# The experts' first product by a Strassen scheme on two of the three channel blocks, with VectorE adding the products up

## The reference

```python
# y: result of a linear recurrence over 768 steps (attention part), as (3072 tokens, 384)
h = y @ w_in                     # 384 -> 2048
g = where(h >= 1, h, where(h <= -1, 0, (h + 1)**2 / 4))
x = g @ w_out                    # 2048 -> 384
P = exp(x @ w_gate - max)        # 3072 tokens x 8 experts
for _ in range(8):               # Sinkhorn: rows, then columns
    P /= P.sum(1) + 1e-9; P /= P.sum(0) + 1e-9; P *= N / E
out = 0
for e in range(8):
    h = maximum(x @ w1[e], 0)    # 384 -> 1024
    out += P[:, e:e+1] * (h @ w2[e])   # 1024 -> 384
```

## Time and profile before

| | |
|---|---|
| median of 3 runs | 2408.18 us (2406.64 to 2408.28) |
| the profiled execution | 2405.71 us, its span 2403.9 us |
| PE busy | 2293.7 us, 95% of the span |
| VectorE busy | 1032.8 us, 43% |
| ScalarE busy | 763.2 us, 32% |
| GpSimd busy | 327.4 us, 14% |
| experts' stage | from 795.1 us to the end |
| second product (L1254 to L1256) | 4608 matmuls of 384 columns |
| first product (L1138 to L1140, tile w_h) | 3456 matmuls of 512 columns |
| mean DMA rate | 44 GB/s |

### The profile page before, as it was taken

How to read it: one execution, slowest core, us unless ns; L and a number is a source line. 1 busy time by engine, 2 the same in 40 slices (tenths; PEclk the granted TensorE clock), 3 DMA queues, 4 the chain that set the end, 5 groups by cost and what they waited for, 6 DMA issues and landing times.

```text
span 2403.9 us, 36292 instructions
## 1 busy us (share of the span) xinstructions
PE 2293.7 (95%) x14011; PEld 2138.7 (89%) x14011; DVE 1032.8 (43%) x2075; ACT 763.2 (32%) x1519; POOL 327.4 (14%) x421
## 2 busy tenths in 40 slices
PE   2689999999999999999999999999999999999999
PEld 2689999999999889999998999999999899999998
DVE  6888888888873343222222222222222222222222
ACT  3455555555545212221122211222112221122211
POOL 0000000000002212111111111111111111111100
PEclk9799999999999999999999999999999999999999
DMA  3211111111111301101111111141011111011101
GB/s 105 83 40 50 50 51 48 48 48 47 48 34 58 132 29 36 36 30 29 31 36 36 29 29 31 36 153 30 30 31 36 36 31 29 29 36 35 29 14 27
DMA packets 95411, 106.63 MB, mean 44 GB/s; under 512 B 9448, under 2 KB 89576, under 8 KB 95208
## 3 DMA queue, kind: packets, MB, share of 16 engines
q1 hardware_dynamic: 95208, 103.99, 14.1%
HBM read 89.80 MB, written 14.16 MB: 43 GB/s over the span
## 4 chain that ended last, share of the span: by engine, by line
PE 82%; DVE 8%; ACT 7%; issue 2%; DMA 1%; SPq 0%; POOL 0%; ACTq 0%; DVEq 0%
PE bank L1138 14%; PE bank L1139 13%; PE bank L1140 13%; PE bank L1254 11%; PE bank L1256 11%; PE bank L1255 11%; PE bank L1119 2%; PE bank L1125 2%; PE bank L1124 2%; PE bank L1129 1%; ACT ubuf L561 1%; ACT ubuf L563 1%; ACT ubuf L559 1%; PE bank L1114 1%; DVE tmp L712 1%
## 5 line engine op out<-in xcount | busy, mean ns | idle before, releaser
L658 ACT ACTIVATE h_h<-bank 128x512 fp32r<-128x512 f32 x384 | 229.5, 598 | 1246.2 <-PE bank L1140 1236.1
L1254 PE MATMUL bank<-w_h,h_h 128*128 128x384 f32 x1536 | 516.4, 336 | 0.0
L1256 PE MATMUL bank<-w_h,h_l 128*128 128x384 f32 x1536 | 516.2, 336 | 0.0
L1255 PE MATMUL bank<-w_l,h_h 128*128 128x384 f32 x1536 | 516.1, 336 | 0.0
L989 DVE SCALAR_TENSOR_TENSOR h_l<-bank,h_h 128x512 fp32r<-128x512 f32 x384 | 264.6, 691 | 519.7 <-ACT h_h L658 519.3
L487 POOL TENSOR_TENSOR w_l<-stage,w_h 128x256 fp32r<-128x256 f32 x384 | 285.0, 744 | 1292.2 <-ACT w_h L639 1292.1
L1138 PE MATMUL bank<-x2h,w_h 128*128 128x512 f32 x1152 | 451.5, 392 | 2.6 <-issue 2.3
L1139 PE MATMUL bank<-x2l,w_h 128*128 128x512 f32 x1152 | 451.7, 392 | 0.0
L1140 PE MATMUL bank<-x2h,w_l 128*128 128x512 f32 x1152 | 448.9, 390 | 0.0
L1002 DVE SCALAR_TENSOR_TENSOR acc<-bank,prob,acc 128x384 f32<-128x384 f32 x168 | 103.9, 618 | 578.9 <-PE bank L1256 578.9
L1254 PEld LDWEIGHTS bank<-w_h,h_h 128*128 128x128 f32 x1536 | 288.1, 188 | 1.9
(11 more groups left out here) (135 smaller groups left out, 2741.4 us busy)
## 6 DMA issues: line engine op xcount, KB each, us to landing
stage<-w_ SPq DMA_DIRECT2D x384, 128.0 KB, 2.1
qb<-q_in_ SPq DMA_DIRECT2D x24, 192.0 KB
kb<-k_in_ SPq DMA_DIRECT2D x24, 192.0 KB
vb<-v_in_ SPq DMA_DIRECT2D x24, 192.0 KB
x_hi<-x2h_s SPq DMA_DIRECT2D x36, 128.0 KB, 1.8
x_lo<-x2l_s SPq DMA_DIRECT2D x36, 128.0 KB, 1.8
x2h<-x_hi SPq DMA_DIRECT2D x6, 768.0 KB, 8.2
x2l<-x_lo SPq DMA_DIRECT2D x6, 768.0 KB, 9.7
```

The costliest lines, as they stand in the source:

```text
L658: act.activation(h_h[:, f], hc[f % 3][:], ACT.Relu).then_inc(hh_done, 1)
L1254: pe.matmul(dst, h_h[:, f, t_], w2s[slot][0][:, f], start=f == 0, stop=False)
L1255: pe.matmul(dst, h_h[:, f, t_], w2s[slot][1][:, f], start=False, stop=False)
L1256: mm = pe.matmul(dst, h_l[:, f, t_], w2s[slot][0][:, f], start=False, stop=f == NF2 - 1)
```

## The change

The first product of the experts, h = x @ w1, is computed block by block. In each half q of the hidden dimension (four tiles) two of the three channel blocks are multiplied by a Strassen-Winograd scheme of two by two blocks; the tokens of a chunk are cut into two columns of 256. It takes seven products where the plain form takes eight; the third channel block takes its plain four, added in the same banks. That makes 11 block products per half, each two tiles by 256 tokens. The banks then hold partial products that have to be added: VectorE makes seven sums per half (`add`, from `p1_s`, `u2_s`, `u4_s`, `u3_s`), three of them to SBUF and four back into the bank. ScalarE copies p1 to SBUF (`keep_p1`), and the Relu and low part read the summed banks.

The scheme needs sums of weight blocks (S_1 to S_4) and of token blocks (T_1 to T_4, D_3). VectorE makes them from the raw tiles (`w1_sums`, `xt_sums`), ScalarE rounds them, and VectorE makes all low parts of w1 and x2's sums (`w1_lo`, `xt_lo`). GpSimd keeps only w2's low parts, in four pieces of 768 elements.

The tokens are taken in three passes of two chunks, not two of three, so that each expert's weights are loaded three times. w1 has one buffer in two halves and two staging tiles; w2 has two buffers. The y banks are two instead of four, and the y block's tiles come in the order 2, 3, 0, 1. The Sinkhorn rounds are cut into `sink_rows` and `sink_columns` and placed in the first two groups. `gate` of the last group stands behind the first four products of group 0. In the tail ahead of the experts VectorE and ScalarE also build the first weights and the first chunk's sums.

```diff
-            expert_lo(0, 0, 0, PER_E)
-            expert_lo(1, 1, 0, PER_E)
+            w2_lo(0, 0)
...
+            def xt_sums(ps, j):
...
+                dve.wait_ge(x2_in[j], 32 * (ps + 1))
+                for a, b in ((T_1, X_11), (T_3, T_3), (T_2, X_22), (T_4, X_21)):
+                    dve.tensor_tensor(to[:, a], high[:, b], low[:, b], ALU.add).then_inc(xt_sum, 1)
...
+            def w1_sums(ex, q):
...
+                dve.tensor_tensor(to[:, S_1], raw_[:, 0, :, 1], raw_[:, 1, :, 1], ALU.add).then_inc(w1_sum, 1)
+                dve.tensor_tensor(to[:, S_3], raw_[:, 0, :, 0], raw_[:, 0, :, 1], ALU.subtract).then_inc(w1_sum, 1)
...
+            def w1_lo(ex, q):
...
+                dve.tensor_tensor(w1l[:, q, W_11:W_22], raw_[:, :, :, 0], w1h[:, q, W_11:W_22].bitcast(F32),
+                                  ALU.subtract).then_inc(w1_low, 1)
...
+                if m == 1:
+                    w1_sums(0, 0)
+                    xt_sums(0, 0)
+                if m == 2:
+                    w1_lo(0, 0)
+                if m == 4:
+                    xt_lo(0, 0)
+                    w1_sums(0, 1)
+                if m == 6:
+                    w1_lo(0, 1)
...
+            def add(g, name, product, kept):
+
+                n = g * len(SUM)
+                q = int(name[3])
+                dve.wait_ge(h2_step, g * len(H2) + H2[product])
+                if name[:2] == "u2":
+                    dve.wait_ge(p1_kept, g * 2 + q + 1)
+                else:
+                    dve.wait_ge(sum_done, n + SUM[{"u4": "u2", "u3": "u2", "22": "u3", "12": "u4", "11": "u2",
+                                                   "21": "u3"}[name[:2]] + name[2:]])
+                dve.tensor_tensor(group_sum(name), pairs_of(h_bank[product]), kept[:], ALU.add).then_inc(sum_done, 1)
...
+            def group(ex, j, ps, e, nxt, x2_next):
+                g = ex * GP + j
+                first, second = (isinstance(g, int) and g == i for i in range(2))
+                build = nxt and j == 1
+                if second:
+                    sink_rows(4)
+                sums(g, 0, ("u2", "u4", "u3", "22", "12"))
+                if second:
+                    sink_columns(4)
+                h_lo(g, "22_0")
+                sums(g, 0, ("11",))
+                h_lo(g, "12_0")
+                if first:
+                    gate_out(GROUPS - 1)
+                    gate_max(0)
+                sums(g, 0, ("21",))
+                h_lo(g, "11_0")
+                if second:
+                    sink_rows(5)
+                sums(g, 1, ("u2",))
+                h_lo(g, "21_0")
...
+                h_lo(g, "11_1")
+                h_lo(g, "21_1")
+                if first:
+                    sink_rows(0)
+                if second:
+                    sink_rows(6)
+                if build:
+                    w1_sums(ex + 1, 0)
+                for k in range(B):
+                    if first:
+                        sink_columns(k)
+                        if k < 3:
+                            sink_rows(k + 1)
+                    if second and k < 2:
+                        sink_columns(6 + k)
+                        if k == 0:
+                            sink_rows(7)
+                    if build and k < 2:
+                        w1_lo(ex + 1, k)
+                    if build and k == 0:
+                        w1_sums(ex + 1, 1)
+                    add_expert(g, j, k, ps, e)
+                    if x2_next and k == 2:
+                        xt_sums(*x2_next)
+                if x2_next:
+                    xt_lo(*x2_next)
...
+            def product(name, j, terms):
+
+                q = int(name[3])
+                for i in range(2):
+                    to = h_bank[name][:, i * HT:(i + 1) * HT]
+                    for n, (w, x) in enumerate(terms):
+                        mm = three(to, (w1h[:, q, w, i], w1l[:, q, w, i]), (x2s[j][0][:, x], x2s[j][1][:, x]),
+                                   n == 0, n == len(terms) - 1)
+                mm.then_inc(h2_step, 1)
...
+                if first:
+                    pe.wait_ge(xt_low, 2 * (ps * GP + j + 1))
+                if not zero:
+                    pe.wait_ge(sum_done, back + SUM["u3_1"])
+                product("p1_0", j, ((W_11, X_11),))
+                if not zero:
+                    pe.wait_ge(hl_done, (g - 1) * len(LOW) + LOW["12_1"])
+                product("p6_0", j, ((S_2, T_2),))
+                product("p5_0", j, ((S_1, T_1),))
+                if not zero:
+                    pe.wait_ge(hl_done, (g - 1) * len(LOW) + LOW["11_1"])
+                product("p7_0", j, ((S_3, T_3), (W_23, X_32)))
+                if zero:
+                    pe.wait_ge(x2l_done, KT * GROUPS)
+                    pe.wait_ge(lg_done, GROUPS - 1)
+                    gate(GROUPS - 1)
+                else:
+                    pe.wait_ge(hl_done, g * len(LOW))
+                if one:
+                    sum_of_columns(4)
+                product("12_0", j, ((S_4, X_22), (W_13, X_32)))
+                pe.wait_ge(p1_kept, g * 2 + 1)
+                product("11_0", j, ((W_12, X_21), (W_13, X_31)))
+                pe.wait_ge(sum_done, here + SUM["u2_0"])
+                product("21_0", j, ((W_22, T_4), (W_23, D_3)))
...
+                pe.wait_ge(sum_done, here + SUM["u3_0"])
+                product("p1_1", j, ((W_11, X_11),))
+                pe.wait_ge(hl_done, g * len(LOW) + LOW["12_0"])
+                product("p6_1", j, ((S_2, T_2),))
...
+                for k, m in enumerate(M_ORDER):
+                    if k >= 2:
+                        pe.wait_ge(acc_done, g * B + k - 1)
...
+                        if n == 4 and (zero or one and k < 2):
+                            sum_of_columns(k if zero else 6 + k)
```

More of the change, by code:

```diff
@@ L378, in _ @@
+            for j in range(GP):
+                sp.wait_ge(out_done[j], PASSES * 16 * B)
         @block.gpsimd
@@ L670, in _, with keep_p1 @@
-            for hf in range(2):
-                e0 = E * hf
-                expert(e0, 0, True)
+            def keep_p1(g, q):
+                act.wait_ge(h2_step, g * len(H2) + H2[f"p1_{q}"])
+                if q:
+                    act.wait_ge(sum_done, g * len(SUM) + SUM["11_0"])
+                elif not isinstance(g, int) or g:
+                    act.wait_ge(sum_done, (g - 1) * len(SUM) + SUM["11_1"])
+                act.activation(p1_s[:], pairs_of(h_bank[f"p1_{q}"]), ACT.Copy).then_inc(p1_kept, 1)
@@ L673, in _, with expert @@
+            def expert(ex, slot, ps, last=False):
+                for j in range(GP):
+                    zero = isinstance(ex, int) and ex == 0
+                    x2_next = (0, 1) if zero and j == 0 else (ps + 1, j) if last and ps + 1 < PASSES else False
+                    group(ex, j, slot, zero and j == 0, not last or ps + 1 < PASSES, x2_next)
+            for ps in range(PASSES):
+                e0 = E * ps
+                expert(e0, 0, ps)
                 with act.Fori(0, 3) as r:
-                    expert(e0 + 1 + 2 * r, 1, True)
@@ new lines, in sums, with h_lo @@
+            def sums(g, q, names):
+                product = {"u2": "p6", "u4": "p5", "u3": "p7", "22": "p5", "12": "12", "11": "11", "21": "21"}
+                kept = {"u2": p1_s, "u4": u2_s, "u3": u2_s, "22": u3_s, "12": u4_s, "11": p1_s, "21": u3_s}
+                for n in names:
+                    add(g, f"{n}_{q}", f"{product[n]}_{q}", kept[n])
+            def h_lo(g, name):
+                dve.wait_ge(hh_done, g * len(SPLIT) + SPLIT[name])
+                dve.scalar_tensor_tensor(tiles_of(h_l, name), group_sum(name), 0.0, tiles_of(h_h, name).bitcast(F32),
@@ new lines, in expert @@
+            def expert(ex, ps, e, last=False):
+                for j in range(GP):
+                    zero = isinstance(ex, int) and ex == 0
+                    x2_next = (0, 1) if zero and j == 0 else (ps + 1, j) if last and ps + 1 < PASSES else False
+                    group(ex, j, ps, e, not last or ps + 1 < PASSES, x2_next)
+            for ps in range(PASSES):
+                e0 = E * ps
+                expert(e0, ps, None)
+                if ps == 0:
+                    for i in range(GP * B):
+                        j, m = i // B, M_ORDER[i % B]
+                        dve.wait_ge(acc_done, i + 1)
+                        dve.tensor_scalar(acc[:, j * B + m], acc[:, j * B + m], prob[:, j * B + m, 0:1], None, ALU.mult)\
+                           .then_inc(scaled, 1)
+                    dve.wait_ge(scaled, GP * B)
@@ L1219, in expert_block, with sum_of_columns, h_block @@
+            def sum_of_columns(r):
+                pe.wait_ge(sink, 3 + 9 * r + 5)
+                pe.matmul(sk[:, 0:E], ones[:], cold[:], start=True, stop=True).then_inc(sink_pe, 1)
+            def h_block(ex, j, ps, first):
+                g = ex * GP + j
+                zero, one = (isinstance(g, int) and g == i for i in range(2))
```

(10 more changed lines are left out.)

498 lines of the change are left out of this document (305 added, 193 removed).

## The result

| | before | after |
|---|---|---|
| median of 4 runs each | 2408.23 us (2406.64 to 2408.81) | 2392.72 us (2389.88 to 2393.52) |
| ratio | | 0.9935, interval 0.9917 to 0.9952 |
| profiled execution, its span | 2405.71, 2403.9 us | 2392.51, 2390.7 us |
| experts' third group (group 2) starts at | 866.23 us | 884.19 us |

The change saves 15.5 us. I had forecast 2380 us, a gain of 28. Group 2 here is the third of the 48 groups, counted from 0: the first after both opening groups. From it to the last matmul lie 46 groups, in both kernels. Before they took 2399.3 - 866.2 = 1533.1 us, after 2386.0 - 884.2 = 1501.8. So the steady part gives 31.3 us, and the start takes 18.0 back: 13.3 us together, as the spans say (2403.9 - 2390.7 = 13.2). The other 2 us of the medians lie outside the spans.

The account below looks back on a forecast made before the run. TensorE's stream of columns was taken to bound the experts' stage. 880.1 + 46 x 32.13 (1478.0) + 5 + 3 + 5 + tail 4.6 gave a 2375.7 us span, forecast as 2380 us, range 2354 to 2410 (8 in 10).

Parts of the forecast that it names:

- case (d): Whole kernel: TensorE sets the time, with only short stalls, as forecast at 2380 us; chance 0.65.
- third tile: Second y block of each expert: third tile waits for the first accumulation, booked at 0.2 us x 24 experts, 5 us.
- Part 1: Experts' h block: 132 matmuls of 256 columns at 116 ns, 15.31 us; a group 32.13 us, 1.16 less.
- Rival (c): Experts' blocks: 256 columns always cost 118 ns and y 177: +18 us, 2398, still faster; chance 0.10.
- Part 2: Experts' h block: VectorE's sums and low parts finish about 0.5 us before TensorE needs them; no stall booked.
- Rival (a): Experts' h block: VectorE sets the pace; at 0.83 us per operation TensorE waits 48 us, 2428, slower; chance 0.13.
- Part 3: Second y block of each expert: VectorE's weight build delays TensorE by 0.2 us x 24 experts, 5 us (0 to 24).
- Rival (b): Third y tile: the weight build holds it up in full, 1 us x 24: +19 us, about 2401; chance 0.12.
- Part 5: Experts' loop, three passes for two: nine loop edges, not six, cost 5 us; x2's sums cost 3 us.
- Passes: Pass changes: x2's sums end 3.7 us into the next h block, 0.8 us of stall, 4 times, 3 us.
- Part 4: Opening two groups: 18 us of stalls, group 0 starting at 793.5 us and group 2 at 880.1, not 866.2.
- theory A: Forecast for e4: matmul pace depends on both operands lying in upper memory, so even groups stay at 120 ns.

Follow-up runs that it names:

- e1: Kernel before the change, each 512-column matmul of the experts' first product cut into two of 256 columns: 2436.61 us, ratio 1.0117.
- e7: Changed kernel, second and third matmul of each triple of the first product cut from 256 to 128 columns, leaving out some low-part terms: 2381.0 us, one run.
- e5: Changed kernel with one more, unused VectorE sum of 512 elements in the first half of every group: 2399.89 us, one run.
- e6: Changed kernel with two more, unused VectorE sums of 512 elements in the first half of every group: 2441.93 us, one run.
- e3: Changed kernel with VectorE's first y accumulation moved ahead of the second half's weight sums: 2389.55 us, ratio 0.9917.
- e2: Changed kernel with the loops over the middle experts written out on all five engines: 2380.32 us, ratio 0.9885.
- e9: Changed kernel with GpSimd starting the second expert's w2 low parts only after the seventh Sinkhorn round: 2394.06 us, ratio 0.9945.
- e4: Changed kernel with the first chunk's x2 buffer laid 43,008 bytes per partition higher, same instructions: 2392.42 us, one run.

## Why the prediction was right in kind and short in size

The time fell inside the range and on the side forecast, by the mechanism forecast, the forecast's case (d). The gain was 15.5 us, not 28. The predicted span was 2375.7 us and the measured one 2390.7, so the sum was 15.0 us short. Term by term, over 46 groups:

```
h block     (15.686 - 15.312) x 46                        +17.2
y block     (16.645 - 16.82) x 46                          -8.0
third tile  0.18 x 23 for 5 booked                         -0.9
loop edges  9.8 for 5 booked                               +4.8
passes and the rest of the steady part, 0.6 for 3 booked   -2.4
start       884.2 for 880.1                                +4.1
tail        4.7 for 4.6                                    +0.1
sum                                                       +14.9
```

That it is no more than 15 is partly luck: the y block and the pass changes erred the other way, by 10.4 us together.

- **Part 1, columns: the mechanism right, the size off.** The step "the 117.8 held in the longer stretch; I take 116" failed. I took a value between two cadences of another stage. Here no steady group runs at 113.3: it is 117.8 with one chunk's x2 and 119.9 with the other's, and e1 shows 117.8 and 119.9 for the same form outside the scheme. 119.9 was above my end of 118. The claim that nearly nothing is fixed, half of 227 to 229 ns, was wrong by 4 to 6 ns, and over 132 x 46 matmuls that is the largest error of the sum. The y block erred the other way: 173.4 ns in every group, so the mean of the earlier trace rows's two kinds was too high. Rival (c) was right on h and wrong on y.
- The gap of the Trainium skill ("TensorE: Matmul & The Clock Gate", Back-to-back issue gap), 81 ns at 128 columns and 131 at 512, isn't seen here: e7's triples, mostly of 128 columns, still take 113 ns a matmul, and 512 columns take 227 to 229.
- **Part 2, VectorE in the h block: right.** The walk gave a lead of about 0.5 us at three products; the trace has 0.64, 0.63 and 0.54, and e5 and e6 price it from the other side: one more operation is all but free, the second costs its whole length. Rival (a) was one operation away.
- **Part 3, the build: right.** 0.2 us booked, 0.18 measured, and e3 removes it. Rival (b), the full microsecond, didn't come.
- **Part 5, loop edges: a wait was missed.** I scaled the edge's own cost with the number of edges (three rounds have two edges between them, so it was six in place of four, not nine in place of six; the ratio is the same). TensorE's own stop is 0.7 to 1.2 us at each of six edges, but VectorE crosses its edge too, some 2.5 us late at four of them, and since part 2 it has 0.6 us of lead. So what nothing waited for before is now waited for. I had both numbers' kinds in hand and didn't join them. e2 shows it: with the edges gone, 10.5 us go.
- **Passes: over-booked.** 3 us for x2's sums behind a pass change; the h blocks at groups 15 and 31 are about 0.16 us longer.
- **Part 4, start: the list right, the sizes mixed.** Booked and measured: `x2l_s` 2 us and 1.97 (4.80 less 2.83); rows in group 0 3.3 and 4.77; group 1's front 4.6 and 3.78; Sinkhorn between group 1's sums 2.3 and 1.21; rows 6 3.4 and 2.43; the build 3.1 and 0.44. Not on the list: 1.18 for `gmax`, since the last gate now stands inside group 0 and its largest value goes through VectorE's queue. Within the two groups the clock fell three times, not two. By the windows it took 5.5 x 0.50 + 7.3 x 0.23 + 7.0 x 0.24 = 6.1 us for 3.4 booked: a stop of 2.4 to 4.8 us costs about two more. And group 0 starts at 794.4, not 793.5: behind the `x2l_s` stop too the granted clock is 0.50, from 763 to 768 us, where before that lasted 3.4 us. These pieces don't explain the whole: the two groups took 89.8 us, 3.2 more than booked, though the stops and the clock inside them come to 19.9 us for 21.1 booked. Some 4 us are spread over the groups without a stop of their own, and their cause is open. The rows in group 0 were 1.5 us longer than booked, for a cause that I hadn't considered: GpSimd and VectorE hold each other up. e9 shows it, by taking GpSimd away and later bringing it back.
- The Trainium skill says it ("SBUF — State Buffer", Who interferes with whom): the two engines share a port pair. VectorE's operations with two SBUF inputs meet a GpSimd operation that reads SBUF; `tensor_scalar` can run in a mode that takes both ports, and then whoever issues first holds the pair for the whole instruction; `tensor_reduce` never meets it. The rows agree: `tensor_scalar` and the two-input operations stretch to 1.52 to 2.31 us, near GpSimd's 1.81 for one operation (7.24 / 4), while the reduction (0.50) and the reciprocal (0.30) beside them keep their length. I had read that GpSimd loses w1 as relief, and hadn't asked where its remaining w2 low parts fall.
- **What lies around the span.** I had added 2.5 us because the median of before stood that far above its profiled execution. After's median stands 0.2 above its own. That is 2.3 us the other way, and leaves 12.7 between 2380 and 2392.7.

**Still open:** why the same 256-column matmul costs 117.8 ns with one chunk's operand and 119.9 with the other's, and 113.3 in a stretch of the stage before. In e1 it goes with the expert's slot, in after with the chunk's buffer. e4 speaks against the distance as far as one move can. What theory A needs, both operands in the upper part, was not tested by itself, and in e1 the even experts, whose weights lie at the high addresses, are the faster ones. It is worth 2 ns x 132 x 23 = 6 us.

## What to carry to other kernels

Price a new matmul shape by the worst cadence that the trace shows for it, and ask how far it lies above the shortest spacing that the trace shows for the narrowest ones, here 0.11 us: a scheme that trades multiplications for narrower matmuls comes close to it, and part of its gain stays there (0.71 us of 1.42 a group here, by e1). When an edit takes an engine's lead down to one operation, every place where that engine starts late (loop edges, pass changes, the start) becomes a wait of the engine that sets the time; write those places out or keep a second operation of lead. And of two vector engines that work at the same time, look at which instructions overlap, not only at their busy shares.

## What the runs showed of the hardware that I hadn't expected

- 256-column matmuls with a weight load each run at 117.8 to 119.9 ns, triples of 256, 128 and 128 columns at 113: from 256 to 171 columns on average the time falls by 4 to 6% only.
- A GpSimd operation of 1.8 us beside it makes a VectorE operation of 0.18 us last 1.70.
- VectorE's first sum came 2.5 us late behind a loop edge (four of six edges), TensorE's own stop there was 0.98 us.
- After the same stop of 3.78 us the 1.2 GHz level lasted 31 us with e7's narrower matmuls, all of them without a pause, and some 3.4 us in after (0.23 of 7.3 us, doubled).
